# Pooled rows of v made by TensorE instead of VectorE, and a first token tile whose value products and inverse roots are made by halves

## The reference, cut to what matters

```python
# attention on q, k, v of [4 batches, 8 heads, 576 rows, 64]
q_d, k_d, v_d = mean over each 4 rows         # 144 "coarse" rows a head
out_d = softmax(q_d @ k_d.T / 8) @ v_d        # coarse attention, per head
out_up = repeat(out_d, 4, axis=2)
# fine attention: only |i - j| < 4 is kept, a band of 7 keys a row
out_local = softmax(masked(q @ k.T / 8)) @ v
x = (out_up + out_local) -> [2304 tokens, 512]
# first feed-forward: root-mean-square norm, then silu(x@w_gate)*(x@w_val) @ w_out, 1536 wide
xn = x / sqrt(mean(x*x) + 1e-6) * rms_g
# second: s*relu(x@w_in)^2 + b, then @ w_out, 2048 wide
```

## Time and profile before

| | us |
|---|---|
| median of 3 runs (lowest, highest) | 980.24 (979.86, 981.27) |
| the profiled execution, its own time | 984.85 |
| its span, first to last instruction | 982.9 |
| TensorE busy in the span | 949.1 (97%) |
| VectorE busy | 537.4 (55%) |
| ScalarE busy | 354.0 (36%) |
| GpSimd busy | 368.4 (37%) |
| mean granted clock of TensorE, as a share of the full one | 0.978 |

### The profile page before, as it was taken

How to read it: one execution, slowest core, us unless ns; L and a number is a source line. 1 busy time by engine, 2 the same in 40 slices (tenths; PEclk the granted TensorE clock), 3 DMA queues, 4 the chain that set the end, 5 groups by cost and what they waited for, 6 DMA issues and landing times.

```text
span 982.9 us, 13208 instructions
## 1 busy us (share of the span) xinstructions
PE 949.1 (97%) x5008; PEld 766.3 (78%) x5031; DVE 537.4 (55%) x813; ACT 354.0 (36%) x816; POOL 368.4 (37%) x192
## 2 busy tenths in 40 slices
PE   7888899989999999999999999999999999999998
PEld 4677699756777777777778998888888888888897
DVE  6888997886775765564542224444433443343343
ACT  2448854752324232422241444222322322222232
POOL 4757866777783876465600454000000000000000
PEclk9898799999999999999999999999999999999999
DMA  9898673433331331012003341102001100100010
GB/s 244 217 259 253 180 216 94 147 87 104 97 111 35 86 106 48 15 38 70 19 9 120 130 129 64 43 1 86 1 1 43 43 0 1 65 1 1 1 43 22
DMA packets 54379, 79.42 MB, mean 81 GB/s; under 512 B 9836, under 2 KB 37068, under 8 KB 52908
## 3 DMA queue, kind: packets, MB, share of 16 engines
q1 hardware_dynamic: 52284, 71.53, 24.8%
q10 hardware_dynamic: 2032, 7.05, 1.9%
HBM read 67.05 MB, written 11.50 MB: 80 GB/s over the span
## 4 chain that ended last, share of the span: by engine, by line
PE 78%; DVE 6%; DMA 4%; POOL 3%; ACT 3%; issue 2%; SPq 2%; ACTq 0%; DVEq 0%; POOLq 0%
PE bank L782 23%; PE bank L922 7%; PE bank L923 7%; PE bank L924 7%; PE bank L905 7%; PE bank L906 7%; PE bank L904 7%; PE bank L818 4%; PE bank L816 4%; PE bank L817 4%; POOL prod L551 3%; DMA rawv<-in_v_dram 2%; ACT prod_a L578 1%; DMA vs<-in_v_dram 1%; PE bank L726 1%
## 5 line engine op out<-in xcount | busy, mean ns | idle before, releaser
L551 POOL TENSOR_TENSOR prod<-qs,ks 128x896 f32<-128x896 f32 x80 | 177.7, 2244 | 89.7 <-DVE sc L596 62.9
L565 POOL TENSOR_TENSOR prod<-sc,vs 128x896 f32<-128x896 f32 x72 | 136.7, 2001 | 64.8 <-DVE x L606 32.7
L945 DVE SCALAR_TENSOR_TENSOR r<-bank,r 128x512 f32<-128x512 f32 (+1 forms) x80 | 51.1, 638 | 181.0 <-ACT r L933 181.0
L906 PE MATMUL bank<-y_h,w2i_l 128*128 128x512 f32 (+1 forms) x320 | 117.7, 368 | 0.0
L933 ACT ACTIVATE r<-bank 128x512 f32<-128x512 f32 (+1 forms) x80 | 44.4, 555 | 181.9 <-PE bank L906 181.2
L838 DVE TENSOR_TENSOR bank<-bank,u 128x512 f32<-128x512 f32 (+1 forms) x66 | 39.6, 599 | 118.0 <-PE bank L782 113.0
L782 PE MATMUL bank<-x_h,wv_h 128*128 128x512 f32 (+1 forms) x264 | 100.0, 390 | 0.0
L596 DVE TENSOR_REDUCE sc<-prod 128x14 f32<-128x896 f32 x80 | 85.7, 1078 | 18.0 <-POOL prod L551 18.0
L816 PE MATMUL bank<-h_h,wo_h 128*128 128x512 f32 (+1 forms) x264 | 93.1, 353 | 0.0
L818 PE MATMUL bank<-h_h,wo_l 128*128 128x512 f32 (+1 forms) x264 | 92.6, 351 | 0.0
L817 PE MATMUL bank<-h_l,wo_h 128*128 128x512 f32 (+1 forms) x264 | 92.5, 351 | 0.0
(11 more groups left out here) (142 smaller groups left out, 1935.7 us busy)
## 6 DMA issues: line engine op xcount, KB each, us to landing
raww<-in_moe_w_out_dram SPq DMA_DIRECT2D x14, 512.0 KB, 4.1
ks<-in_k_dram SPq DMA_DIRECT2D x16, 280.0 KB
vs<-in_v_dram SPq DMA_DIRECT2D x16, 280.0 KB, 5.0
y_scr<-y_st ACTq DMA_DIRECT2D x4, 1024.0 KB, 5.7
raww<-in_moe_w_in_dram SPq DMA_DIRECT2D x8, 512.0 KB, 3.5
y_raw<-y_scr SPq DMA_DIRECT2D x4, 1024.0 KB, 4.8
out_dram<-o_st SPq DMA_DIRECT2D x16, 256.0 KB, 2.8
rawq<-in_q_dram SPq DMA_DIRECT2D x3, 1152.0 KB, 15.2
```

The costliest lines, as they stand in the source:

```text
L551: pool.tensor_tensor(dst, qv, kv, ALU.mult).then_inc(prod_ready, 1)
L565: pool.tensor_tensor(dst, pv, vv, ALU.mult).then_inc(prod_ready, 1)
L906: last = pe.matmul(o, w2i_l[:, m, kk, :], y_h[t % 2][:, kk, 0:w], start=False, stop=kk == DT - 1)
```

## The change

Pooled v. For each batch the four rows are now added by TensorE: a unit "v" of `turn_pooled` does four matmuls of the identity with the four strided slices of the loaded rows (72 rows by 512 columns, float32), accumulated in `CTR`, and ScalarE copies the sum into `dv`. There are two such units a batch, 8 units a batch in all, so units stand after the heads 2 to 27 (before: 5 to 10, 12 to 17, 20 to 25). All batches are loaded with 72 partitions in two halves; `pool_v0`, `pool_v`, `store_vd`, `load_dv` and the DRAM tensor `v_scr` go. Batches 1 to 3 share two buffers, so a load of batch 2 or 3 waits for TensorE's unit of the batch before.

Halves. GpSimd makes the value steps of tile 0 in the order even n, then odd n; two steps q times k of tile 1 come ahead of them. The v windows of tile 0 get eight buffers (`vs3`) instead of four. `inverse_root0` is called once for each pair of columns (2 columns each), the first before the last coarse heads, the second after the second step of the first block. What belongs to the second pair (value steps 9, 11, 15, the add, the squares, the root) stands behind the last coarse head on VectorE and ScalarE. `inverse_root_of` and the waits count one root more.

```diff
-UNIT0 = [("q", 0), ("k", 0), ("q", 1), ("k", 1), ("q", 2), ("k", 2)]
-UNIT = [("q", 0), ("q", 1), ("k", 0), ("k", 1), ("q", 2), ("k", 2)]
+UNIT0 = [("q", 0), ("k", 0), ("q", 1), ("k", 1), ("q", 2), ("k", 2), ("v", 0), ("v", 1)]
+UNIT = [("q", 0), ("q", 1), ("k", 0), ("k", 1), ("v", 0), ("q", 2), ("k", 2), ("v", 1)]
+QK0 = 6
-UNIT_FROM = {1: 5, 2: 4, 3: 4}
+UNIT_FROM = 4
-PRODUCTS = [("qk", 0, n) for n in range(16)] + [("pv", 0, n) for n in range(16) if n not in ACT_PV[0]] + [("qk", 1, n) for n in range(16)]
+PRODUCTS = [("qk", 0, n) for n in range(16)] + [("qk", 1, 0), ("qk", 1, 1)]
+HALVES = [n for half in range(2) for n in range(half, 16, 2)]
+PRODUCTS += [("pv", 0, n) for n in HALVES if n not in ACT_PV[0]] + [("qk", 1, n) for n in range(2, 16)]
...
 def slot_units(n):
+    if n in (2, 3):
+        return ((0, QK0 + n - 2),)
+    b, i = divmod(n - UNIT_FROM, UNITS)
+    return ((b + 1, i),) if 0 <= b < B - 1 else ()
...
 def weight_hi(act, n):
             if n == FIRST_ORDER.index(("out", 0)):
                 act.wait_ge(cpv, HEADS)
+                act.wait_ge(prod_ready, pv_at(0, 15) + 1)
+                act.wait_ge(act_made, len(ACT_PV[0]))
 def weight_lo(eng, n):
             if n < SLOTS:
-                eng.wait_ge(v_pooled[1], 1)
-                eng.wait_ge(v_pooled[3], 1)
+                eng.wait_ge(ctr_ps, UNITS * B)
...
+        def inverse_root0(dve, pair):
+            dve.wait_ge(sq_ready, 2 * pair + 2)
+            a_link(dve, dve.tensor_scalar(smax[:, 0:2], sqs[:, 2 * pair:2 * pair + 2], 1.0 / E, 1e-6, ALU.mult, ALU.add))
+            inverse_root(dve, smax, 2 * pair, 2)
...
+            def load_rawv(b, g):
+                rows = v_rows[b][:, H * g:H * (g + 1), :]
+                if b == 0:
+                    sp.dma_start(rawv0[0:JH, H * g:H * (g + 1), :], rows).then_inc(rawv0_loaded[g], 16)
+                    return
+                if b > 1:
+                    sp.wait_ge(ctr_ps, UNITS * (b - 1) + UNIT.index(("v", g)) + 1)
+                sp.dma_start(rawv[1 + g][0:JH, :, :], rows).then_inc(rawv_loaded[g], 16)
             sp.wait_ge(consts_made, 3)
             load_qk(sp, 0, 0)
-            load_rawv0(0)
+            load_rawv(0, 0)
+            load_qk(sp, 0, 1)
             load_rawq(1)
-            load_qk(sp, 0, 1)
+            load_rawv(0, 1)
             load_qk(sp, 0, 2)
-            load_rawv0(1)
             load_rawk(1)
             load_qk(sp, 0, 3)
-            load_rawv(1)
+            load_rawv(1, 0)
             load_qk(sp, 0, 4)
+            load_rawv(1, 1)
             load_qk(sp, 0, 5)
             load_rawq(2)
-            load_dv(sp, 1)
             load_rawk(2)
...
     # scalar: copy of a v unit
+                if kind == "v":
+                    wait(act, cpv, H * (b - 1))
+                    act.activation(dv[0:JH, b % 2, H * g:H * (g + 1), :], CTR[0:JH, :].rearrange("p (h d) -> p h d", d=D), ACT.Copy).then_inc(ctr_evac, 1)
...
     # vector, behind the last coarse head
             least(31)
-            qk_reduce(dve, 1, 1)
-            exponent_sums(3, 1)
-            qk_reduce(dve, 1, 2)
             dve.wait_ge(small_loaded, 48)
             split_lo(dve, 0, 0)
             split_lo(dve, 0, 1)
-            qk_reduce(dve, 1, 3)
+            exponent_sums(3, 1)
+            pv_reduce(dve, 0, 9)
+            pv_reduce(dve, 0, 11)
+            pv_reduce(dve, 0, 15)
+            add_pooled0(dve, 1)
             weight_lo(dve, 3)
             weight_lo(dve, 2)
+            qk_reduce(dve, 1, 2)
+            hidden_mul(dve, 0)
             weight_lo(dve, 4)
-            hidden_mul(dve, 0)
             finish_pooled(3, 0)
             hidden_lo(dve, 0)
+            qk_reduce(dve, 1, 3)
             qk_reduce(dve, 1, 4)
             finish_pooled(3, 1)
             qk_reduce(dve, 1, 5)
             hidden_mul(dve, 1)
             weight_lo(dve, 6)
             hidden_lo(dve, 1)
+            inverse_root0(dve, 1)
             hidden_mul(dve, 2)
...
     # tensor: a v unit, and the wait of the value products
+                if kind == "v":
+                    pe.wait_ge(rawv0_loaded[g], 16)      # b == 0; else rawv_loaded[g], 16 * b
+                    pe.wait_ge(ctr_evac, n)
+                    rows = rawv0[0:JH, H * g:H * (g + 1), :] if b == 0 else rawv[1 + g][0:JH, :, :]
+                    for f in range(FAC):
+                        last = pe.matmul(CTR[0:JH, :], ident[0:JH, 0:JH], rows[:, :, f * D:(f + 1) * D], start=f == 0, stop=f == FAC - 1)
+                    last.then_inc(ctr_ps, 1)
...
-                    if b == 0 and h % 4 == 0:
-                        pe.wait_ge(v0_pooled, h // 4 + 1)
-                    if b and h == 0:
-                        pe.wait_ge(dv_loaded[b % 2], 16 * ((b + 1) // 2))
+                    if h % 4 == 0:
+                        pe.wait_ge(ctr_evac, UNITS * b + (UNIT if b else UNIT0).index(("v", h // 4)) + 1)
```

More of the change, by code:

```diff
@@ L240, in build @@
         at = [gl_start]
-        rawv = [None] + [place(at, f"rawv{b}", [P, QT, FAC * D], F32) for b in (1, 3)]
+        rawv = [None] + [place(at, f"rawv{g}", [P, H, FAC * D], F32) for g in range(2)]
+        at = [gl_start + 2 * QT * FAC * D * 4]
         vs2 = place(at, "vs2", [P, 2, WIN * D], F32)
@@ L319, in build @@
         qk_loaded = [sem(f"qk_loaded{i}") for i in range(WSLOTS0)]
-        v_loaded = [sem(f"v_loaded{i}") for i in range(WSLOTS0)]
+        v_loaded = [sem(f"v_loaded{h}") for h in range(H)]
         prod_ready, prod_used = sem("prod_ready"), sem("prod_used")
@@ L520, in load_v @@
         def load_v(sp, a, h):
-            last = before_in_slot(a, h)
+            last = v_before(a, h)
             if last is not None:
@@ L673, in squares, with inverse_root @@
                                accum_out=sqs[:, 4 * part + f:4 * part + f + 1]).then_inc(sq_ready, 1)
[L675 to L680, removed]
+        def inverse_root(dve, scratch, f0, count):
+            var, newt, root = [scratch[:, i * FAC:i * FAC + count] for i in range(3)]
+            half, rin = halfv[:, f0:f0 + count], rinv[:, f0:f0 + count]
+            dve.tensor_scalar_mul(half, var, -0.5)
+            dve.tensor_scalar(rin.bitcast(I32), var.bitcast(I32), -0.5, float(RSQRT_BITS), ALU.mult, ALU.add)
             a_link(dve, dve.tensor_scalar(root.bitcast(I32), var.bitcast(I32), -0.5, float(RSQRT_BITS), ALU.mult, ALU.add))
             for n in range(NEWTON):
[L683 to L684 removed]
+                a_link(dve, dve.tensor_tensor(newt, root, rin, ALU.mult))
+                a_link(dve, dve.tensor_tensor(newt, newt, half, ALU.mult))
                 if n < NEWTON - 1:
[L686 to L687 removed]
+                    dve.scalar_tensor_tensor(out=root, in0=newt, scalar=1.5, in1=rin, op0=ALU.add, op1=ALU.mult)
+                last = dve.scalar_tensor_tensor(out=rin, in0=newt, scalar=1.5, in1=rin, op0=ALU.add, op1=ALU.mult)
                 if n < NEWTON - 1:
@@ L1265, in exponents @@
                                    accum_out=csum[0:JH, b % 2, 2 * h + a, 0:1]).then_inc(cexp, 1)
-            for i in range(UNITS):
+            for i in range(QK0):
                 keep_pooled(0, i)
@@ L1439, in _ @@
             squares(act, 1, 1)
-            normalise(act, range(FAC), 2)
+            normalise(act, range(FAC), 3)
             hidden_hi(act, 15)
@@ L1469, in _ @@
                     if m == 9:
-                        normalise(act, range(FAC), 1 + c)
+                        normalise(act, range(FAC), 2 + c)
                 if (c, m) in ROUND_AT and ROUNDS[c + 1] > 2:
@@ L1865, in turn_pooled @@
                     else:
-                        last = pe.transpose(to, qd[:, 3 * g + t, :] if kind == "q" else kd[:, 0, 3 * g + t, :], ident[:, :])
+                        last = pe.transpose(to, qd[:, 3 * g + t, :] if kind == "q" else kd[:, 3 * g + t, :], ident[:, :])
                 last.then_inc(ctr_ps, 1)
-            for i in range(UNITS):
+            for i in range(QK0):
                 turn_pooled(0, i)
                 if i % 2:
-                    keep_running(CSC[0], 3 if i < UNITS - 1 else 2)
+                    keep_running(CSC[0], 3 if i < QK0 - 1 else 2)
             for n in range(HEADS + VAL_LAG):
```

226 lines of the change are left out of this document (99 added, 127 removed).

## The result

The changed kernel takes 1021.66 us (median of 4 runs, 1017.81 to 1023.99), the kernel before 980.75 beside it (4 runs): ratio 1.0409, 95% interval 1.0368 to 1.0449, so 4.1% slower. The forecast of 987.8 had the sign and a fifth of the size. The profiled execution took 1020.22 us with a span of 1018.4, 35.5 more than before. By the medians the change costs 41 us: the profiled execution of the kernel before was 4.6 us above its median, and no trace shows where in it those 4.6 us lie. The first gate starts at 148.27 instead of 122.69, + 25.6; from there to the end it takes 870.1 instead of 860.2, + 9.9.

What follows compares the result with a forecast made beforehand. It took TensorE, busy 97%, as the bound, so the first gate's start mattered; + 3.6 us to the gate and + 4.0 behind it gave + 7.6, 984.85 to 992.5 profiled, median 987.8, range 973 to 998.

Steps and rivals of the forecast that it cites:

- The unit: Four float32 matmuls over 512 columns on TensorE: 3.5 us at the full clock, 6.8 at the lower.
- Unit v(0,1): Behind head 3, waiting for the second half of v, landing at 27: taken as 5.1 us, head 4 at 32.8.
- Head 31 to the gate: Last coarse head to first gate matmul: 6.5 us with the full clock and x ready, against 10.8 before.
- the 3.6 of the forecast: Delay of the first gate matmul: 126.3 instead of 122.7 us.
- the path of TensorE, walked at the full clock: Head stage up to the first gate, summed head by head with units and 3 us of waits: gate at 126.3.
- rival A: Head stage: v units buy back slow-clock stretches worth 14.5 us, the freed queue helps; total 974, chance 0.26.
- Rival B: Head stage: the clock falls as often as before, slow units or heads around them add 8 us; 996, chance 0.12.
- TensorE is late next: Before the first gate: the 16.6 us taken from VectorE buy nothing, since TensorE then sets the gate.
- D: Before the gate: the halves shorten nothing, as TensorE's heads decide and not x; costs nothing by itself.
- the freed queue buys nothing: Head stage: SP's freed queue brings loads earlier, but not past the pace of the heads.
- by one pass the change would gain: The v units on TensorE: with one pass a unit would be 0.9 us and the change would gain.
- The mechanism and the slack: Behind the gate: 8.1 us more on VectorE, less 1.9 of slack, stalls TensorE 6.2 us; net + 4.0.

Runs made afterwards that it cites:

- wait_filled: f32_burst_wait with 27 bf16 dummies (6 us) ahead of its wait, so that TensorE is busy while it waits: 993.6 us against 1002.4.
- the bare blocks: Kernel before plus eight TensorE blocks, 28 us in all, without new waits or loads: 988.0 us with bf16 dummies, 989.6 with float32 matmuls.
- whole_v_dve: Kernel before with v added by VectorE straight into the layout of the values, no detour through DRAM, no halves: 986.2 us, ratio 1.0023 to 1.0081.
- q_one_slice: Changed kernel with each v unit doing one of its four matmuls: 997.4 us, ratio to the kernel before 1.0142 to 1.0213.
- the v part alone: Kernel before with only the v change, second half of v loaded early, one of four matmuls a unit: 983.4 us, ratio 1.0002 to 1.0051.
- low_twice: Kernel before with VectorE computing the low parts of weight pieces 3, 2, 4 and 6 twice: 986.1 us, ratio 1.0031 to 1.0071.
- v_early: Changed kernel with the load of the second half of v of batch 0 right behind the first half's: 1014.2 us, ratio 1.0313 to 1.0398.
- f32_burst_wait: Kernel before plus eight float32 blocks, the one behind head 3 waiting for the second half of v of batch 0: 1002.4 us, ratio 1.0148 to 1.0255.

## Why the prediction was wrong

The steps in its own order, against the trace after:
- The unit: 3.5 forecast, 3.60 to 3.65 measured at the full clock. Right. The Trainium skill, "FP8 and Floating Point Precision", section TensorE Precision Notes, says that true float32 takes four passes; the estimate of 3.4 worked out from it agrees with the trace.
- Unit v(0,1) starts at 27.09 (27 forecast), but takes 7.10, not the 5.1 taken between 3.5 and 6.8: head 4 at 35.27 instead of 32.8, + 2.5.
- Head 9 at 58.68 instead of 52.8: + 3.4 more, since the clock stayed low until 42 us.
- Heads 9 to 17 took 24.4 us, and 8 x 1.69 + 6 x 0.66 + 2 x 3.5 = 24.5 was the forecast's sum for them: exact where the clock held.
- Heads 9 to 28: 72.8 instead of 58.9, + 13.9. The waits in it are 2.28 + 1.50 + 1.28 + 0.45 + 1.05 = 6.6 us, and the clock was 0.54 to 0.55 from 93 to 108 us, 15 x 0.46 = 6.9.
- Waits, 3 us forecast on top, are in the row above: - 3.0. Head 28 to 31: 5.1, as forecast. Head 31 to the gate: 11.7 instead of 6.5, + 5.2, with waits of 2.58 and 1.05 us and the lower clock again.
- Sum, with the 3.6 of the forecast first: 3.6 + 2.5 + 3.4 + 13.9 - 3.0 + 5.2 = 25.6, the measured delay of the gate.

The step that failed is "the path of TensorE, walked at the full clock". The walk held the low clock in one unit only, with 1.6 us. Measured, the clock to the gate was 0.86: over the 117.1 us in which TensorE was busy that is about 0.14 x 117.1 = 16.4 us, 14.8 more than the walk had. Idle time was 15.2 us instead of the walk's 7.7, 7.5 more. Together 22.3, for the 22.0 us between the forecast's delay of the gate and the measured one. In the kernel before the same two numbers are 0.15 x 90.0 = 13.5 us and 17.0 us. So the walk counted on getting most of both back, and the change got back almost nothing: the eight units, 28.8 us at 3.6 each, went into the path nearly whole.

The rows for it were there: the kernel before also had 0.85 in this stretch, and the argument took its slow stretches as something that the added matmuls would end (rival A), where they begin behind waits, and the change adds waits. Rival B named the fall, but priced it at 8 us, with a chance of 0.12. The Trainium skill, "TensorE: Matmul & The Clock Gate", section What's actually happening, has the slow clock as the default, with activity lifting it; wait_filled agrees, and the forecast read from it only that more work helps, not that a wait ahead of long work can double the time of that work.

Right were: that TensorE is late next (the bare blocks, with no wait of their own, moved the gate by 5.4 us in bf16 and 9.7 in float32), and that the halves shorten nothing (D); but D's "costs nothing by itself" is not borne out: by the estimates above they cost 1 to 7 us before the gate. That the freed queue buys nothing was not tested by itself: in whole_v_dve the 34.8 us of waits for `v_scr` are gone, but the queue waits 44.0 us for products and low parts instead of 25.7, and VectorE is busy 7.5 us more. Wrong was "by one pass the change would gain": with a quarter of the unit it does not (q_one_slice 997.4, the v part alone 983.4). Rival A's 14.5 us for the slow stretches counts idle moments too; by TensorE's busy time in the earlier trace rows it is 13.3.

Behind the gate + 9.9 instead of + 4.0. The mechanism and the slack were right (low_twice), the size was not (and 8.9 less 0.9 is 8.0, not 8.1). The second pair on VectorE took 3.2 us for the reduces and 1.0 waiting for GpSimd, 1.9 for the add and 3.9 for the root (169.15 to 173.05), 10.0 instead of 6.8, and the low parts among them stretched to 3.1 us. TensorE's waits were 10.9 us up to tile 1 instead of 6.2. At tile 1 the wait of 2.19 us for the scaled x is gone, as forecast. The kernel before had another there, of 1.70 us for the low parts of x (at 225.47), and in the kernel after this one takes 1.96 (at 256.24); all waits at tile 1 fell from 4.8 to 2.3 us. 10.9 - 2.6 = 8.3 of the 9.9 us are waits; an estimate of 0.8 to 1.0 us more is the clock, which fell behind two of these waits (3.27 and 1.96 us) where it fell behind one before (2.19).

## What to carry to other kernels

A chain walked instruction by instruction must be walked at the clock that its waits leave it. Here waits of 3.5 us and more ahead of a long float32 unit made 3.6 us into 7, and one of 6 us cost more by that than by itself. No safe length of a wait comes out of these traces. In the kernel after, waits of 1.39, 1.28 and 1.05 us (at 48.6, 113.7 and 127.8) left the clock at 1.00. But in the kernel before it fell behind two close together of 1.53 and 0.34 us (at 69 to 70), and in v_early a unit behind a wait of 1.05 us took 4.97.

Before work moves to an engine that has idle time, ask whether the idle time is one's own slack or a wait for the engine that is being relieved: 20 us less work on VectorE came back as 42 us more of waiting for scores. Where a late operand can't be brought forward, harmless matmuls in the wait are worth trying, but only on an engine that sets the pace: they gave 8.9 us beside the bare blocks, 3.2 in the changed kernel (not clear of noise), and nothing in the kernel before.

## What the runs showed of the hardware

Six us of extra matmuls made a program 8.9 us faster (wait_filled against f32_burst_wait). And VectorE's time for one and the same shape depends on what runs beside it. Low parts of 128x1024 on VectorE in the kernel before, then GpSimd's products beside them:

```profile
122.83 3.12 DVE L428 TENSOR_TENSOR wg_l<-raww,wg_h 128x1024 bf16<-128x1024 f32 x1
125.88 1.21 DVE L428 TENSOR_TENSOR wo_l<-raww,wo_h 128x1024 fp32r<-128x1024 f32 x1
...
163.82 1.22 DVE L428 TENSOR_TENSOR wg_l<-raww,wg_h 128x1024 bf16<-128x1024 f32 x1
```

```profile
117.69 7.18 POOL L551 TENSOR_TENSOR prod<-qs,ks 128x896 f32<-128x896 f32 x3 [0.24 <-DVE sc L596]
130.51 11.31 POOL L551 TENSOR_TENSOR prod<-qs,ks 128x896 f32<-128x896 f32 x4 [5.64 <-DVE sc L596]
```

The first took 3.12 us while GpSimd multiplied (until 124.9), the second 1.21 while it was idle (until 130.5). The type of the result is not the reason: the third, of the same form as the first, took 1.22 with GpSimd idle from 162.4 to 168.6. Nor does each one beside GpSimd take long: the one at 121.59 took 1.32. The Trainium skill, "Perfetto Trace Analysis", section Optimizing Scalar/DVE Operations, says that the two share a read port; the trace agrees. Durations from one order of work, as those of the second pair here, don't hold in another.
